# Attention and two gated layers in one kernel: sums at layer boundaries on VectorE, a new order for second groups and the first loads

## The reference

```python
scores = q @ k^T / sqrt(64) - slope[h] * |i - j|      # only 0 <= i - j < 128, else masked
attn   = softmax(scores) @ v                          # per batch and head
x      = attn as (2304, 512)
x      = (sigmoid(x @ w_gate) * (x @ w_val)) @ w_out  # first layer, inner width 1536
out    = ((x @ w1) * (x @ w2)) @ w3 @ w_out2          # second layer, inner width 1024
```

## Time and profile before

| | before |
|---|---|
| median of three runs | 958.38 us (953.91 to 958.84) |
| the profiled execution | 958.44 us, span 956.7 us |
| TensorE (PE) busy | 916.2 us, 96% |
| GpSimd (POOL) busy | 633.2 us, 66% |
| VectorE (DVE) busy | 543.3 us, 57% |
| ScalarE (ACT) busy | 455.5 us, 48% |
| mean granted TensorE clock | 0.989 of 2.4 GHz |

### The profile page before, as it was taken

One profiled execution on the slowest core, in us unless ns is written; L12 is line 12 of the kernel. 1 busy time (PEld: TensorE's weight loads), 2 busy tenths in 40 slices (PEclk: granted clock), 3 DMA queues, 4 the chain that ended last, 5 costly groups with the idle time before them and its releaser, 6 DMA issues. The chain is left out here.

```text
span 956.7 us, 15336 instructions
## 1 busy us (share of the span) xinstructions
PE 916.2 (96%) x5272; PEld 796.1 (83%) x5272; DVE 543.3 (57%) x1261; ACT 455.5 (48%) x999; POOL 633.2 (66%) x507
## 2 busy tenths in 40 slices
PE   6999989999998999999999997999999999989998
PEld 3444578888887889988888886888988999979998
DVE  3445455655655565766556656556655555554554
ACT  3446375655453643466554554544535333334430
POOL 2227588566746876778766656786769966658940
PEclk9999999999998999999999999999999999999999
DMA  7454323122212222141223201320132112212201
GB/s 238 124 164 144 120 83 117 61 83 83 95 42 62 85 75 77 56 148 54 91 86 101 85 27 46 110 96 23 45 111 88 66 67 70 72 37 78 78 23 66
DMA packets 46140, 80.75 MB, mean 84 GB/s; under 512 B 4208, under 2 KB 27376, under 8 KB 46064
## 3 DMA queue, kind: packets, MB, share of 16 engines
q1 hardware_dynamic: 46064, 79.77, 25.4%
HBM read 72.94 MB, written 6.82 MB: 83 GB/s over the span
## 5 line engine op out<-in xcount | busy, mean ns | idle before, releaser
L562 PE MATMUL quad_ps<-xs_hi,wq_hi 128*128 128x384 f32 x840 | 296.4, 353 | 11.9 <-ACT s L783 9.8
L564 PE MATMUL quad_ps<-xs_hi,wq_lo 128*128 128x384 f32 x840 | 283.9, 338 | 0.0
L563 PE MATMUL quad_ps<-xs_lo,wq_hi 128*128 128x384 f32 x840 | 283.7, 338 | 0.0
L562 PEld LDWEIGHTS quad_ps<-xs_hi,wq_hi 128*128 128x128 f32 x840 | 159.7, 190 | 32.5 <-issue 18.8
L1115 POOL TENSOR_TENSOR soft<-soft,recip 128x512 f32<-128x512 f32 (+2 forms) x80 | 74.2, 928 | 162.1 <-DVE recip L893 162.1
L562 PE MATMUL o_ps<-h_hi,wo_hi 128*128 128x384 f32 x480 | 168.6, 351 | 7.8 <-DVE xf L988 7.3
L564 PE MATMUL o_ps<-h_hi,wo_lo 128*128 128x384 f32 x480 | 162.2, 338 | 0.0
L563 PE MATMUL o_ps<-h_lo,wo_hi 128*128 128x384 f32 x480 | 161.9, 337 | 0.0
L563 PEld LDWEIGHTS quad_ps<-xs_lo,wq_hi 128*128 128x128 f32 x840 | 159.9, 190 | 0.0
L564 PEld LDWEIGHTS quad_ps<-xs_hi,wq_lo 128*128 128x128 f32 x840 | 159.6, 190 | 0.0
L1166 POOL TENSOR_TENSOR wq_lo<-wsum,wq_hi 128x1024 fp32r<-128x1024 f32 x60 | 143.4, 2389 | 8.2 <-POOL wq_lo L1159 0.9
(11 more groups left out here) (57 smaller groups left out, 1300.3 us busy)
## 6 DMA issues: line engine op xcount, KB each, us to landing
raw_q<-w SPq DMA_DIRECT2D x24, 512.0 KB, 3.5
raw_q<-w_gate SPq DMA_DIRECT2D x18, 512.0 KB, 3.5
raw_q<-w_val SPq DMA_DIRECT2D x18, 512.0 KB, 4.5
wo_lo_raw<-w_out SPq DMA_DIRECT2D x18, 512.0 KB, 3.7
wo_lo_raw<-w_times_wout SPq DMA_DIRECT2D x12, 512.0 KB, 3.7
w_sb<-w3t SPq DMA_DIRECT2D x16, 256.0 KB, 3.1
q_sb<-qT SPq DMA_DIRECT2D x16, 192.0 KB, 4.1
bias<-bias SPq DMA_DIRECT2D x12, 256.0 KB, 3.9
```

Source lines behind the costliest of these rows:

```text
L562: pe.matmul(out, lh, rh, start=start, stop=False, skip_group_check=onto)
L563: pe.matmul(out, lh, rl, start=False, stop=False, skip_group_check=onto)
L564: return pe.matmul(out, ll, rh, start=False, stop=stop, skip_group_check=onto)
```

## The change

It has these parts. All x sums and nearly all x rests go to VectorE at the boundary from first to second layer (GpSimd keeps the rest of P1; at the boundary to the next third it makes the rests of P1, P3 and P2), in a new order among the `add_up` calls, and ScalarE's `x_hi` calls are reordered to match; P4's comes only in the following gate. `sums_lo` of the second half of a first group's weights moves from its gate up into pair0. In a second group `weights_hi(g, 1)` moves on ScalarE behind `keep` and the exponentials, `plain_lo`, `sums_lo` and `out_lo` of the group before on GpSimd in front of `weight_sums` and `normalise`. SP issues the loads for these weights one or two sections earlier. The products in pair0 and pair1 finish tiles sooner. In the head, folds begin in slot 1, the queries' buffers are not cleared any more (TensorE reads only the rows that are there), SP starts at once and ScalarE's queue issues the first queries and bias.

```diff
--- before.py
+++ after.py
@@ -47,2 +47,4 @@
 JOBS_TO = [sum(job[0] < t for job in JOBS) for t in range(NPASS + 1)]
+
+FIRST_HALF = [STEPS_TO[1] - 4, STEPS_TO[2] - 3, STEPS_TO[3]]
 HEAD = STEPS_TO[1]
@@ -76,7 +78,12 @@
 
-    return 3 + k // 2 if k < 50 else 28 + (k - 50) // 3
+    return 1 + k * 27 // 44 if k < 44 else 28 + (k - 44) // 5
+
+
+def by_slot(slots):
 
+    return {s: [i for i, at in enumerate(slots) if at == s] for s in slots}
 
-FOLDS_IN = [[k for k in range(NFOLD) if fold_slot(k) == s] for s in range(SLOTS + 1)]
-W3_LOAD_SLOT = {fold_slot(4 * h - 9): h for h in range(3, HALVES)}
+
+FOLDS_IN = by_slot([fold_slot(k) for k in range(NFOLD)])
+W3_LOAD_SLOT = by_slot([fold_slot(4 * h - 9) if h >= 3 else -1 for h in range(HALVES)])
 COPY_SLOT = {fold_slot(IB * m + IB - 1) + 1: m for m in range(IB - 1)}
@@ -395,3 +402,4 @@
                 third = inst // 2
-                eng.wait_ge(x_ready, STEPS_HALF[third] if j in (P1, P5) else STEPS_TO[third + 1])
+                eng.wait_ge(x_ready, STEPS_HALF[third] if j in (P1, P5) else FIRST_HALF[third] if j == P2
+                            else STEPS_TO[third + 1])
 
@@ -464,4 +472,2 @@
                 wait(sp, o_done, tiles_to(g - 2))
-                if g == 0:
-                    sp.wait_ge(fold_half, HALVES)
                 if r < G1:
@@ -484,6 +490,3 @@
 
-            sp.wait_ge(zeroed, 1)
             load_k(0)
-            load_q(0)
-            load_bias(0)
             load_w3(0)
@@ -497,4 +500,4 @@
             load_v(0)
-            load_w3(1)
             load_wo2(4)
+            load_w3(1)
             load_wo2(5)
@@ -508,3 +511,3 @@
             load_bias(1)
-            for s in range(SLOTS):
+            for s in range(SLOTS + 1):
                 for j in range(3, HEAD_JOBS + 2):
@@ -515,4 +518,4 @@
                         load_v(j)
-                if s in W3_LOAD_SLOT:
-                    load_w3(W3_LOAD_SLOT[s])
+                for hf in W3_LOAD_SLOT.get(s, ()):
+                    load_w3(hf)
                 for u in (2, 3, 4):
@@ -525,10 +528,16 @@
                     load_quad(0, 1)
-            store_fold(IB - 1)
+            load_quad(1, 0)
             for sec, (g, kind) in enumerate(SECTIONS):
                 if kind == "gate":
-                    if g + 1 < NG:
+                    if first_of(g):
+                        load_quad(g + 1, 1)
+                    elif g + 1 < NG:
                         load_quad(g + 1, 0)
                     load_out(g)
-                if kind == "val" and g + 1 < NG:
+                if g == 0 and kind == "gate":
+                    store_fold(IB - 1)
+                if kind == "val" and not first_of(g) and g + 1 < NG:
                     load_quad(g + 1, 1)
+                if kind == "pair1" and g + 2 < NG:
+                    load_quad(g + 2, 0)
                 for j in range(HEAD_JOBS + 2, len(JOBS)):
@@ -576,3 +585,4 @@
                     pe.wait_ge(x_ready, n if drained else n - 1)
-                keys, q = keys_of(n), slice(i * P, (i + 1) * P)
+                m = rows_of(n)
+                keys, q = keys_of(n), slice(i * P, i * P + m)
                 first = JOBS[j][3] + (i - 1) * P - key_base(j)
@@ -582,3 +592,3 @@
                     rows = slice(h * D, (h + 1) * D)
-                    mm = pe.matmul(score_bank(n, h)[:, keys], q_sb[st][rows, q], k_sb[st][rows, where],
+                    mm = pe.matmul(score_bank(n, h)[0:m, keys], q_sb[st][rows, q], k_sb[st][rows, where],
                                    start=True, stop=True)
@@ -699,3 +709,3 @@
                     turn(s - LAG_TURN)
-                for k in FOLDS_IN[s]:
+                for k in FOLDS_IN.get(s, ()):
                     fold(k)
@@ -703,4 +713,2 @@
                     scores(s)
-            for k in FOLDS_IN[SLOTS]:
-                fold(k)
             for sec, (g, kind) in enumerate(SECTIONS):
@@ -722,4 +730,5 @@
                         lo = 4 * (kind == "pair1")
-                        parts = [(lo + k, of) for k, of in ((0, g - 1), (1, g - 1), (0, g), (1, g),
-                                                            (2, g - 1), (3, g - 1), (2, g), (3, g))]
+                        order = (0, 1, 0, 1, 2, 2, 3, 3) if lo == 0 else (0, 0, 1, 1, 2, 2, 3, 3)
+                        half = (0, 0, 1, 1, 0, 1, 0, 1) if lo == 0 else (0, 1, 0, 1, 0, 1, 0, 1)
+                        parts = [(lo + k, g - 1 + of) for k, of in zip(order, half)]
                     for i, (k, of) in enumerate(parts):
@@ -791,3 +800,2 @@
                 if g == 0 and blk == C11:
-                    act.wait_ge(fold_stored, 16 * IB)
                     act.wait_ge(pv_done, HEAD)
@@ -803,2 +811,4 @@
 
+            nc.scalar.dma_start(q_sb[0][:, 0:queries(0)], qT[0, :, 0:queries(0)]).then_inc(q_in[0], 16)
+            nc.scalar.dma_start(heads(bias[0]), bias8[0:2].rearrange("h p c -> p h c")).then_inc(bias_in[0], 16)
             act.wait_ge(small_set, 1)
@@ -818,3 +828,5 @@
                     weights_hi(0, 1)
-            for j in (P6, P2, P7, P3, P4):
+                if s == 30:
+                    x_hi(0, P2)
+            for j in (P6, P7, P3):
                 x_hi(0, j)
@@ -827,10 +839,14 @@
                     keep(2 * g)
-                if kind == "val":
+                    if first_of(g):
+                        x_hi(inst - 1, P4)
+                elif kind == "val":
                     gate(g, C21)
                     keep(2 * g + 1)
+                elif more and kind == "pair1" and g % GP == G1 - 1:
+                    x_hi(inst, P1)
                 if n is not None:
                     exponentials(n)
-                if kind in ("proj", "pair0"):
-                    hidden_hi(g, C21)
                 if kind == "gate":
+                    if g and first_of(g - 1):
+                        weights_hi(g, 1)
                     out_hi(g)
@@ -849,5 +865,4 @@
                     hidden_hi(g, C12)
-                    if first_of(g):
-                        weights_hi(g + 1, 1)
                 elif kind in ("proj", "pair0"):
+                    hidden_hi(g, C21)
                     if more:
@@ -857,8 +872,11 @@
                     if more and g % GP == GP - 1:
-                        x_hi(inst, P1)
-                        x_hi(inst, P5)
+                        for j in (P1, P5, P3, P2, P6):
+                            x_hi(inst, j)
+                elif g % GP == G1 - 1:
+                    x_hi(inst, P5)
+                    if m is not None:
+                        out_copy(m)
+                    for j in (P3, P6, P7, P2):
+                        x_hi(inst, j)
                 else:
-                    if more and g % GP == G1 - 1:
-                        x_hi(inst, P1)
-                        x_hi(inst, P5)
                     if m is not None:
@@ -866,4 +884,3 @@
                     if more:
-                        for j in (P6, P3, P7, P2, P4):
-                            x_hi(inst, j)
+                        x_hi(inst, P7)
 
@@ -919,2 +936,5 @@
                     a, b = b_block(inst, 1, 1), pair_of(xt[0][:, :])
+                elif j == P7:
+                    wait(dve, xs_split[P7], inst)
+                    a, b = b_block(inst, 1, 1), b_block(inst, 0, 1)
                 else:
@@ -976,2 +996,4 @@
                 dve.wait_ge(h_hi_done, 4 * g + blk + 1)
+                if g == 0:
+                    dve.wait_ge(fold_stored, 16 * IB)
                 nc.vector.tensor_tensor(out=h_lo[g % 2][:, piece(blk)], in0=quad[BANK_OUT[blk]][:, 0:TH],
@@ -993,5 +1015,2 @@
             nc.vector.memset(recip[:, 0:1], 0.0).then_inc(small_set, 1)
-            for b in range(3):
-                op = nc.vector.memset(q_sb[b][:, :], 0.0)
-            op.then_inc(zeroed, 1)
             dve.wait_ge(soft_zeroed, 1)
@@ -1010,7 +1029,11 @@
                     x_lo(0, P5)
+                if s == 31:
+                    x_lo(0, P2)
             x_sum(0, P6)
+            x_sum(0, P7)
             x_lo(0, P6)
+            x_lo(0, P7)
             x_sum(0, P4)
+            x_lo(0, P3)
             fold_copy(IB - 1)
-            x_lo(0, P2)
             for sec, (g, kind) in enumerate(SECTIONS):
@@ -1020,7 +1043,8 @@
                     e = project_of(g - 1)
-                if kind == "pair0":
-                    hidden_lo(g, C12)
-                if n is not None:
-                    score(n)
                 if kind == "gate":
+                    if g % GP == G1:
+                        x_lo(inst - 1, P2)
+                        x_lo(inst - 1, P3)
+                    if n is not None:
+                        score(n)
                     if g and first_of(g - 1):
@@ -1030,2 +1054,4 @@
                     sums_26(2 * g)
+                    if first_of(g):
+                        x_lo(inst - 1, P4)
                     if m is not None:
@@ -1067,2 +1097,5 @@
                 elif kind == "pair0":
+                    hidden_lo(g, C12)
+                    if n is not None:
```

(64 more changed lines are left out.)

6 lines of the change are left out of this document (3 added, 3 removed).

## The result

| | before | after |
|---|---|---|
| median of 15 runs each, in turn on one chip | 957.82 us (953.91 to 959.03) | 961.55 us (959.93 to 963.13) |
| ratio, 95% interval | | 1.0047 [1.0037, 1.0058] |
| the profiled execution | 958.44 us, span 956.7 | 960.82 us, span 959.0 |
| mean granted TensorE clock | 0.989 | 0.984 |

The change makes the kernel slower by 0.5%: +3.7 us by the medians, +2.3 us between the two profiled spans, where +6.6 us was forecast (961.55 lies in the range of 951 to 971). It is a small sum of large terms of both signs, so the terms are what has to be read.

What follows compares the result with a forecast made beforehand. TensorE was busy 96% of the span, so gains were only in its waits and half clocks at boundaries and in the head. -3.0 + 0.3 - 3.0 - 6.5 + 14.0 - 4.2 + 9.0 = +6.6 gave 965.0 us, range 951 to 971.

Steps and rivals of the forecast that it cites:

- the case taken for likeliest: Whole kernel: all terms hold, with late turns in four second groups and a held-up next-third boundary; 965.0 us, slower.
- Second groups with attention: Four gates and vals: late cast makes `normalise` and the turn late; +4.4 of waits and +9.6 of half clock, +14.0 us.
- Rival 1: The second groups' turns come in time, so the 14.0 term goes to 0; 951.0 us, faster, chance 0.18.
- rival 2: The second groups' turns are late but the clock holds; -9.6, 955.4 us, the same, chance 0.22.
- Second layer to the next third: Pair0: VectorE's x operations, held by GpSimd's port use, delay `add_up(2)` and tile 4; +9.0 us with half clock.
- Rival 3: VectorE isn't held up at the third's boundary; -9.0, 956.0 us, the same, chance 0.10.
- First to second layer, with attention: Thirds 1 and 2: the 1.50 us wait in pair1 goes, the score wait and its half clock stay; -3.0 us together.
- The same in the last third: Pair1 and gate, without scores: 16.5 us in place of 23.02, half clock included; -6.5 us.
- Second groups, last third: Both, without `normalise`: nothing left to wait for, 16.67 us falls to 14.57 us; -4.2 us.
- Head: Earlier loads and products filling idle time: 2.1 us less idle and an earlier clock rise for some 0.9; -3.0 us.
- the +0.3: Head: six sums in a row on VectorE before section 0 delay the fourth operand; +0.3 us (0 to +1).

Runs made afterwards that it cites:

- Experiment 1: Kernel after with GpSimd's `normalise` moved up right behind `sums_lo` in the gate of every second group; 943.29 us, 0.9863 of before.
- Experiment 2: Kernel after with the second groups' old orders on ScalarE and GpSimd restored; 952.08 us, 0.9963 of before.
- experiment 9: Kernel after with GpSimd waiting for tile 3's `add_up` before its three `x_lo` and `sums_lo` at the boundary to the next third; 961.58 us, 1.0054 of before.
- experiment 8: Kernel after with GpSimd's `x_lo` of P1, P3, P2 and `sums_lo` moved from pair0 to pair1 at the boundary to the next third; 965.06 us.
- experiment 5: Kernel after with `normalise` right behind `sums_lo` and `out_lo` behind `weight_sums` in second groups' gates; 941.53 us, 0.9846 of before.
- experiment 7: Kernel after with the first query and bias loads back on SP behind the first key load and the query clearing; 963.32 us, 1.0071 of before.
- experiment 6: Kernel after with the head's weight products in their old slots, from slot 3, two per slot; 962.40 us, 1.0065 of before.
- experiment 3: Kernel after with VectorE's `add_up` calls ahead of `x_lo(P5)` and `x_sum(P6)` at the boundary to the next third; 951.36 us, 0.9942 of before.
- experiment 4: Kernel after with the score ahead of `x_lo(P2)` and `x_lo(P3)` on VectorE in a second layer's first gate; 955.52 us, 0.9984 of before.
- experiment 10: Kernel after with the edits of experiment 1, experiment 3, experiment 4 and experiment 5 together; 926.87 us, 0.969 of before.

## Why the prediction was right, and where it was off

The waits of the case taken for likeliest (chance 0.40) are what happened; no rival did. By the prediction's own bounds, though, 961.55 is still "the same" (under 963.2) and not "slower", and the sum came this near in part by luck: the terms missed by up to 3.7 us in both directions. Point by point:

- **Second groups with attention.** The mechanism, place and chain of times were right (in the group shown the cast 4.4 us, `normalise` 15.9 us into the gate; waits 3.38, 3.78, 2.19 and 3.27 us where 4.0, 3.4, 2.4 and 3.2 stood). Experiments 1 and 2 show the cause. Half clocks followed all four, as taken. +12.1 for +14.0: mis-sized was the price of a half clock, 2.4 us each. Counted from its gate the turn came 1.1, 1.8, 0.4 and 1.6 us later than before, 4.9 in all for the forecast's 4.4; what stands behind the turn took 1.6, 2.5, 1.5 and 1.6 us longer, 7.2 in all for 9.6. Three of the four half clocks were 3.4 us long and only the second 6.8; the 2.4 is an average over three stretches, two of them long. Rival 1 needed the cast 4 us sooner, rival 2 a clock that holds: neither was so. Experiment 1 had neither and gained 18.3 us because it took `normalise` off the end of the row, which no rival had named.
- **Section before the first of them.** -1.5 where the forecast had no term: the val of the very first group had two waits before, 0.48 us for a gate on ScalarE at 122.27 and 0.79 for `soft` at 125.40, and has neither now. The change makes `sums_lo` of that group already in the head, and the forecast gave that no term. No experiment shows that this is the cause.
- **Second layer to the next third.** +8.1 for +9.0: waits 3.46 and 4.51 us for 3.5 and 4.4; the half clock behind the first is 3.4 us of a busy TensorE, so 1.7 us for the 2.4 taken. Rival 3 (no hold-up) falls with experiment 9.
- **First to second layer, with attention.** The wait of 1.5 us went and that for `negmax` stayed, at 3.07 and 3.26 us, as forecast. -6.0 for -3.0: mis-sized was the score wait, thought to stay as long as it was with its whole half clock. Beside the 0.3 and 0.1 us that it shrank, the half clock near 298 was 6.8 us long and is 3.4 now, and the one near 592 didn't come. That part is chance: behind the same wait of 3.25 us there the run of experiment 8 has one of 6.8 us.
- **The same in the last third.** -5.6 for -6.5. The step that failed is that the last `add_up` ends 0.6 us into the gate; it ends at 861.8, 1.9 us into it, because GpSimd's `weight_sums` hold the port in turn with VectorE's sums (about 1.5 us each in place of 0.95) and `add_up(6)` stood behind them. TensorE waits 1.29 us for P2 in place of 0.3.
- **Second groups, last third.** The step that failed is "nothing is left to wait for". -0.5 for -4.2: the gate still stands for products and weights, and `out_lo` ahead of `weight_sums` makes ScalarE's second cast hold `hidden_hi` (experiment 5).
- **Head.** -3.8 for -3.0, and the +0.3 did not come. The clock is up from 9.6 us on (before: 15.1), read from the products of 128x512, which are shown with some 1.06 us each until then and 0.59 behind it. In the other runs with this head it is up from 9.4 to 12.5 us on, and against the one profiled run of the kernel before the gain is 2.5 to 4.0 us, so the -3.0 lies within what executions differ by. The forecast gave most of it to products that fill the idle time; by experiment 7 the loads carry 1.5 us or more, and by experiment 6 no gain of the slots can be seen.

From +6.6 to +2.8: two gains fell short, by 3.7 and 0.9 us, and the other terms came out better by 3.0, 1.9, 1.5, 1.1 and 0.9. The forecast of 965.0 was 3.45 us above the median.

## What to carry to other kernels

When work is moved on an in-order engine, look at what each call behind it is waited for, and put the one call whose reader is TensorE ahead of calls that serve the next section; here that is one moved `normalise`, and it turns a change that costs 0.5% into one that gains 1.4%. An idle time that repeats pays twice, once itself and once by the clock behind it, so waits of 3 us are worth cutting below 1.8 even where they can't be removed (in these runs no half clock followed an idle time of up to 1.86 us). A call moved to a later section starts as early as before unless something holds it, and a buffer freed later may hold a load on SP, and with it every load queued behind.

## What the runs showed of the hardware

- The granted clock fell behind idle times in a scattered way. Over the profiled runs of the kernel before, the kernel after and experiments 1 to 10, in the stretches behind the start: of 27 idle times of TensorE between 0.9 and 1.86 us none was followed by a half clock; of 11 between 1.92 and 2.7 us nine were (two of the three at 2.22 were not); of 42 between 3.0 and 3.5 us 34 were; of 16 of 3.7 us and more all were, eleven of them for 6.8 us, the others for 3.4. Where TensorE is busy all through a half clock of 3.4 us it loses 1.7 us, and 2.7 in the one of 6.8 near 327. So the same wait of 3.25 us costs 3.3 us in one execution and 5 or more in another. The runs of a kernel with such waits spread more: 953.91 to 959.03 for the kernel before and 959.93 to 963.13 for the kernel after (15 runs each), 925.95 to 927.04 in experiment 10 (4 runs), where none is left.
- At the start the clock rises at different times with the same instructions: in eleven profiled runs with the head of the kernel after at 9.4 to 12.5 us, and the head ends between 108.90 us (rise at 9.4) and 110.40 (rise at 12.4 and 12.5).
- An operation of VectorE with two SBUF inputs that takes 0.95 us alone took up to 2.85 beside a row of GpSimd operations, and GpSimd's grew as well: the same `x_lo` takes 1.86 us alone and 2.5 when VectorE runs beside it. An operation that reads PSUM and SBUF (`add_up`, 0.55 us) kept its time: the 64 of the kernel after that lie wholly beside GpSimd operations take 0.56 us at most.
